# Both products of the first MLP as seven block products in chunks of 768 tokens, with p kept in DRAM between

## What is computed

```python
scores = scale * np.matmul(q, k.transpose(0, 1, 3, 2))          # masked to the window, softmax
x = np.matmul(attn, v)                                          # 2304 x 512
a = x @ w1; b = x @ w2                                          # 512 -> 1024 each
h = a * b @ w3; x = h @ w_out                                   # 1024 -> 1024 -> 512
h = x @ w_in; g = np.maximum(0.01 * h, h); out = g @ w_out2     # 512 -> 2048 -> 512
```

## Time and profile before

| | us |
|---|---|
| median of 3 runs (lowest, highest) | 795.57 (795.39, 797.1) |
| the profiled execution | 795.03 |
| its span, first to last instruction | 793.2 |
| TensorE busy | 775.2 |
| VectorE, ScalarE, GpSimd busy | 406.3, 374.5, 132.8 |
| HBM traffic | 155.74 MB, 195 GB/s over the span |

### The profile page before, as it was taken

The page is one execution under the profiler, slowest core; times in us unless marked ns, Lnnn a source line. Parts: engine busy times, 40 slices in busy tenths (PEclk is TensorE's granted clock), DMA queues, the critical chain, the costliest instruction groups (busy, mean ns, idle before and its releaser), DMA issues. The chain is left out here.

```text
span 793.2 us, 12523 instructions
## 1 busy us (share of the span) xinstructions
PE 775.2 (98%) x4944; PEld 751.5 (95%) x4944; DVE 406.3 (51%) x582; ACT 374.5 (47%) x814; POOL 132.8 (17%) x129
## 2 busy tenths in 40 slices
PE   6999999999999999999999999999999799999998
PEld 5788999999999999999999999999999699999998
DVE  4775442442443343333255577659778555445451
ACT  4775441442442343343235666456668454444441
POOL 0110450542451111111114005105100000000000
PEclk9999999999999999999999999999999999999999
DMA  7976462663563232221602675764999997768731
GB/s 276 325 248 220 159 224 97 230 258 129 208 236 113 86 118 97 83 87 34 239 1 81 237 267 193 265 224 161 359 356 339 321 315 250 217 189 245 212 95 60
DMA packets 65050, 155.74 MB, mean 196 GB/s; under 512 B 5344, under 2 KB 32992, under 8 KB 64992
## 3 DMA queue, kind: packets, MB, share of 16 engines
q1 hardware_dynamic: 55968, 137.12, 51.2%
q10 hardware_dynamic: 9024, 17.83, 5.9%
HBM read 104.07 MB, written 50.86 MB: 195 GB/s over the span
## 5 line engine op out<-in xcount | busy, mean ns | idle before, releaser
L287 PE MATMUL acc<-parts,weights_a 128*128 128x384 f32 x488 | 166.2, 341 | 0.4 <-DVE weights_b L873 0.4
L289 PE MATMUL acc<-parts,weights_a 128*128 128x384 f32 x488 | 163.2, 335 | 0.0
L288 PE MATMUL acc<-parts,weights_a 128*128 128x384 f32 x488 | 163.2, 334 | 0.0
L922 DVE TENSOR_TENSOR parts<-arena,parts 128x768 fp32r<-128x768 f32 x72 | 68.6, 958 | 66.0 <-ACT parts L726 65.9
L726 ACT ACTIVATE parts<-arena 128x768 fp32r<-128x768 f32 x72 | 60.5, 847 | 73.4 <-PE acc L289 25.8
L287 PE MATMUL acc<-weights_b 128*128 128x384 f32 (+1 forms) x256 | 93.3, 364 | 1.6 <-DVE weights_b L873 0.9
L287 PEld LDWEIGHTS acc<-parts,weights_a 128*128 128x128 f32 x488 | 91.7, 188 | 0.8 <-issue 0.8
L288 PEld LDWEIGHTS acc<-parts,weights_a 128*128 128x128 f32 x488 | 91.8, 188 | 0.0
L289 PEld LDWEIGHTS acc<-parts,weights_a 128*128 128x128 f32 x488 | 91.6, 188 | 0.0
L288 PE MATMUL acc<-weights_b 128*128 128x384 f32 (+1 forms) x256 | 90.0, 352 | 0.0
L289 PE MATMUL acc<-weights_b 128*128 128x384 f32 (+1 forms) x256 | 89.9, 351 | 0.0
(11 more groups left out here) (185 smaller groups left out, 1613.1 us busy)
## 6 DMA issues: line engine op xcount, KB each, us to landing
arena<-g_between SPq DMA_DIRECT2D x84, 384.0 KB, 4.1
g_between<-arena SPq DMA_DIRECT2D x24, 960.0 KB, 5.1
arena<-qkm_steps SPq DMA_DIRECT2D x36, 576.0 KB, 4.5
arena<-v_steps SPq DMA_DIRECT2D x36, 256.0 KB, 3.9
g_between<-arena SPq DMA_DIRECT2D x24, 384.0 KB, 6.1
arena<-wprod_tiles SPq DMA_DIRECT2D x16, 512.0 KB, 4.3
weight_sums<-arena ACTq DMA_DIRECT2D x16, 512.0 KB, 3.2
arena<-weight_sums SPq DMA_DIRECT2D x16, 512.0 KB, 5.6
```

Source lines behind the costliest of these rows:

```text
L287: eng.matmul(out_ap, w_hi, m_hi, start=start, stop=False, skip_group_check=resumed)
L288: eng.matmul(out_ap, w_hi, m_lo, start=False, stop=False, skip_group_check=resumed)
L289: return eng.matmul(out_ap, w_lo, m_hi, start=False, stop=stop, skip_group_check=resumed)
L922: dve.tensor_tensor(b[:, BW:2 * BW], t_raw[traw_slot(k)], b[:, 0:BW].bitcast(F32), ALU.subtract).then_inc(t_lo, 1)
```

## The change

The first MLP takes the form of the second. The order on TensorE is now:

- The first stage, with 12 attention steps instead of 6. `hu_sums` on POOL and `split_hu` on ACT and DVE make, in each of the 16 slots, one half of a unit of w1 and w2 with its sums (7 x 128 columns). wsum is copied out of PSUM and stored to DRAM.
- The rounds AB: 12 rounds of 14 slots in the order `AB_SEQ`. A slot (r, i, s) is product i for branch s (s = 0 is a, s = 1 is b), 6 matmuls of 384 columns. p's four blocks are products of two SBUF tensors (`make_p11`, `make_p22`, `make_p12`) or of PSUM and SBUF (`make_p21`); their sums follow (`p_sums`), and three stores take all to `pt_dram`. The other 24 attention steps lie in rounds 0 to 6 (`SCORES`); the values are copied by DVE instead of ACT.
- y: `y_product` for three chunks, seven products of two blocks `ty` each, blocks loaded through a ring of five places (two until k = 8).
- The second MLP as before, at other addresses.

The weight sums of w_in and w_out (`presums`, `load_pre`, `store_pre`) now start behind the last attention step, and their stores are issued by SP. wsum's units are summed and split by DVE and ACT in rounds 9 and 10 (`WSUM_SPLIT`). The mask comes once and not with every step. The diff, cut to its core:

```diff
+AB_SEQ = []
+for _r in range(AR):
+    AB_SEQ += [(_r, P1, 0), (_r, P1, 1)]
+    if _r == 0:
+        AB_SEQ.append((_r, P5, 0))
+    AB_SEQ += [(_r, P5, 1), (_r, P2, 0), (_r, P6, 0), (_r, P6, 1), (_r, P2, 1), (_r, P7, 0), (_r, P7, 1),
+               (_r, P3, 0), (_r, P3, 1), (_r, P4, 0), (_r, P4, 1)]
+    if _r + 1 < AR:
...
+AB_PAIR = (0, 1, 2, 3, 0, 1, 2, 3, 2, 3, 0, 1)
...
+SCORES0 = (-1, 0, 1, 2, 4, 5, 6, 7, 8, 9, 10, 11)
+TURN0, VALUES0 = 2, 3
...
+        SCORES[(_c + 1) * CSTEPS + _j] = slot_of(4 * _c, 2 + (33 * _j + 5) // 10)
+EXPS_A, EXPS_B, RECIP, TURN, VALUES = 2, 3, 4, 5, 8
...
+WSUM_SPLIT = {(9, 3): 0, (9, 8): 1, (10, 4): 2, (10, 9): 3}
+TY_FIRST = {3: 0, 5: 1, 9: 2, 12: 3}
...
+            def store_p(r):
+                c, jj = r // ROUNDS, AB_PAIR[r]
+                sp.wait_ge(p22_done, r + 1)
+                sp.wait_ge(pt3_made, r + 1)
+                sp.dma_start(pt_dram[c, 0:3, :, jj].rearrange("b p t -> p b t"), pa_st[:, :]).then_inc(p_stored[0], 16)
+                sp.wait_ge(pt1_made, r + 1)
+                sp.wait_ge(pt2_made, r + 1)
+                sp.dma_start(pt_dram[c, 3:5, :, jj].rearrange("b p t -> p b t"), pb_st[:, 0:2]).then_inc(p_stored[1], 16)
+            def store_p_late(r):
+                c, jj = r // ROUNDS, AB_PAIR[r]
+                sp.wait_ge(c21_done, 2 * r + 2)
+                sp.wait_ge(pt4_made, r + 1)
+                sp.dma_start(pt_dram[c, 5:7, :, jj].rearrange("b p t -> p b t"), pb_st[:, 2:4]).then_inc(p_stored[2], 16)
             def load_pre(u):
-                if u >= 2:
+                if u < 2:
+                    sp.wait_ge(values_done, NSTEP)
+                    sp.wait_ge(masked, NSTEP)
+                else:
                     sp.wait_ge(pre_stored[u % 2], u // 2 * 16)
-                elif u == 1:
-                    sp.wait_ge(piece_lo, NFIRST)
...
+            def store_pre(u):
+                sp.wait_ge(pre_s3, u + 1)
+                sp.wait_ge(pre_made, u + 1)
+                sp.dma_start(sums_dram[u], pre_raw[u % 2][:, QW:5 * QW]).then_inc(pre_stored[u % 2], 16)
...
+            def load_ty(k):
+                c, i, jp = k // (NPROD * JPY), k // JPY % NPROD, k % JPY
+                if i == 0 and jp == 0:
+                    for n in range(3):
+                        sp.wait_ge(p_stored[n], 16 * ROUNDS * (c + 1))
+                if TEARLY <= k < TEARLY + TRAWY - SPARE:
+                    sp.wait_ge(p_stored[k - TEARLY], 16 * AR)
+                if TY_BEFORE[k] is not None:
+                    sp.wait_ge(ty_lo, TY_BEFORE[k] + 1)
+                sp.dma_start(ty_raw[TY_SLOT[k]].rearrange("p (j t) -> p j t", j=2),
+                             pt_dram[c, P_AT[i], :, 2 * jp:2 * jp + 2]).then_inc(ty_in[TY_SLOT[k]], 16)
...
+                if r > 0 and n == slot_of(r, 2):
+                    store_p(r - 1)
+                    store_p_late(r - 1)
+            for u in range(2):
+                load_pre(u)
+            for r in range(8, AR):
+                store_p(r - 1)
+                store_p_late(r - 1)
+                if r == 8:
+                    load_wsum(0)
+                    load_wsum(1)
+                for u in range(3 * (r - 8), 3 * (r - 8) + 3):
+                    store_pre(u)
+                    load_pre(u + 2)
+                if r == 9:
+                    load_wsum(2)
+                    load_wsum(3)
+                if r == 10:
+                    load_ty(0)
+                    load_ty(1)
+            load_ty(2)
+            load_ty(3)
+            load_ty(4)
+            store_p(AR - 1)
+            load_ty(5)
+            store_p_late(AR - 1)
+            for k in [6, 8, 7] + list(range(9, TBY)):
+                load_ty(k)
+                if k == 8:
+                    store_pre(12)
+                    load_pre(14)
+                if k == 10:
...
+            def hu_sums(h):
+                a11, a12, a22, s4, s2, a21, s1 = [hu_raw[h % 2][:, q * P:(q + 1) * P] for q in range(NPROD)]
+                pool.wait_ge(hu_in[h % 2], 32 * (h // 2 + 1))
+                if h >= 2:
+                    pool.wait_ge(hu_lo, h - 1)
+                pool.tensor_tensor(s1, a21, a22, ALU.add).then_inc(hu_s1, 1)
+                pool.wait_ge(hu_s1, h + 1)
+                pool.tensor_tensor(a21, a11, a21, ALU.subtract).then_inc(hu_s3, 1)
+                pool.tensor_tensor(s2, s1, a11, ALU.subtract).then_inc(hu_s2, 1)
+                pool.wait_ge(hu_s2, h + 1)
+                pool.tensor_tensor(s4, a12, s2, ALU.subtract).then_inc(hu_made, 1)
...
+            def split_wsum(j):
+                act.wait_ge(wu_s3, j + 1)
+                act.wait_ge(wu_made, j + 1)
+                act.wait_ge(prod_done[P4], 2 * (9 + j // 2))
+                act.activation(units[HALF_UNITS + j][:, 0], wsum_raw[j % 2], ACT.Copy).then_inc(wu_hi, 1)
+            def split_ty(k):
+                if k < NPROD:
+                    act.wait_ge(prod_done[k], 2 * AR)
+                else:
...
+                    save_wsum(0)
+                    store_wsum(0)
+                for g in range(CSTEPS):
+                    if SCORES0[g] == k - 1:
+                        exps(g, range(HP))
+                split_hu(k)
...
+            for k in range(TROUND, TBY + NPROD):
+                c, i, step = (k - NPROD) // (NPROD * JPY), (k - NPROD) // JPY % NPROD, (k - NPROD) % JPY
+                r = YR0 + c
+                if k < TBY:
+                    split_ty(k)
+                else:
+                    split_x(NC2, XS_POS[k - TBY])
+                if k in Y_UNIT_SPLIT:
+                    split_unit(Y_UNIT_SPLIT[k])
+                if k >= NPROD and step == JPY - 1:
+                    for s in range(2):
+                        if i == P1:
+                            copy_p1(r, s)
...
+            def make_p11(r):
+                dve.wait_ge(c11_done, 2 * r + 2)
+                if r == 0:
+                    for m in range(2, 4):
+                        dve.wait_ge(wsum_stored[m], 32)
+                else:
+                    dve.wait_ge(p_stored[0], 16 * r)
+                dve.tensor_tensor(pa_st[:, 0], p1_sb[:, 0], p1_sb[:, 1], ALU.mult).then_inc(p11_done, 1)
+            def make_p22(r):
+                dve.wait_ge(c22_done, 2 * r + 2)
+                dve.tensor_tensor(pa_st[:, 2], p5_sb[:, 0], p5_sb[:, 1], ALU.mult).then_inc(p22_done, 1)
+            def make_p12(r):
+                dve.wait_ge(c12_done, 2 * r + 2)
+                dve.tensor_tensor(pa_st[:, 1], u2_sb[:, 0], u2_sb[:, 1], ALU.mult).then_inc(p12_done, 1)
+            def p_sums(r):
+                dve.wait_ge(p11_done, r + 1)
+                dve.wait_ge(p12_done, r + 1)
+                if r == 0:
+                    for m in range(2):
+                        dve.wait_ge(wsum_stored[m], 32)
+                else:
+                    dve.wait_ge(p_stored[1], 16 * r)
+                dve.tensor_tensor(pb_st[:, 0], pa_st[:, 1], pa_st[:, 0], ALU.subtract).then_inc(pt1_made, 1)
+                dve.wait_ge(p22_done, r + 1)
+                dve.wait_ge(pt1_made, r + 1)
+                dve.tensor_tensor(pa_st[:, 1], pa_st[:, 2], pa_st[:, 1], ALU.subtract).then_inc(pt3_made, 1)
+                dve.tensor_tensor(pb_st[:, 1], pa_st[:, 2], pb_st[:, 0], ALU.subtract).then_inc(pt2_made, 1)
+            def make_p21(r):
+                dve.wait_ge(c21_done, 2 * r + 1)
+                dve.wait_ge(prod_done[P4], 2 * r + 2)
+                if r > 0:
+                    dve.wait_ge(p_stored[2], 16 * r)
+                dve.tensor_tensor(pb_st[:, 2], bank(r, P4, 1)[:, 0:CT], p1_sb[:, 0], ALU.mult).then_inc(c21_done, 1)
+                dve.wait_ge(c21_done, 2 * r + 2)
+                dve.wait_ge(pt2_made, r + 1)
+                dve.tensor_tensor(pb_st[:, 3], pb_st[:, 2], pb_st[:, 1], ALU.subtract).then_inc(pt4_made, 1)
+            def wsum_sums(j):
+                a11, a12, a22, s4, s2, a21, s1 = [wsum_raw[j % 2][:, q * QW:(q + 1) * QW] for q in range(NPROD)]
+                dve.wait_ge(wu_in[j % 2], 32 * (j // 2 + 1))
+                dve.tensor_tensor(s1, a21, a22, ALU.add).then_inc(wu_s1, 1)
+                dve.wait_ge(wu_s1, j + 1)
+                dve.tensor_tensor(a21, a11, a21, ALU.subtract).then_inc(wu_s3, 1)
+                dve.tensor_tensor(s2, s1, a11, ALU.subtract).then_inc(wu_s2, 1)
+                dve.wait_ge(wu_s2, j + 1)
+                dve.tensor_tensor(s4, a12, s2, ALU.subtract).then_inc(wu_made, 1)
+            def split_wsum(j):
+                dve.wait_ge(wu_hi, j + 1)
+                u = units[HALF_UNITS + j]
+                dve.tensor_tensor(u[:, 1], wsum_raw[j % 2], u[:, 0].bitcast(F32), ALU.subtract).then_inc(wu_lo, 1)
+            def split_ty(k):
+                dve.wait_ge(ty_hi, k + 1)
+                b = block_places[k % NPROD]
+                dve.tensor_tensor(b[:, BW:2 * BW], ty_raw[TY_SLOT[k]], b[:, 0:BW].bitcast(F32),
+                                  ALU.subtract).then_inc(ty_lo, 1)
...
```

(94 more changed lines are left out.)

1571 lines of the change are left out of this document (847 added, 724 removed).

## The result

The changed kernel takes 893.79 us (median of four runs, 891.6 to 896.06); the kernel before took 795.48 us beside it. The ratio is 1.1233, with a 95% interval of 1.1199 to 1.1267: slower by 12%. The forecast said slower, but by 1.1%. The profiled execution has a span of 891.5 us, so 137.7 us were added to the ideal 753.8 of the forecast, where 49.1 had been expected.

What follows compares the result with a forecast made beforehand. TensorE's instruction count was taken to set the end, with starvation at hand-overs through DRAM. Ideal 753.8 plus 49.1 of stalls gave a span of 802.9, plus 1.8 made 804.7, stated as 804.5 us (1.1% slower), range 785 to 819.

Steps and rivals of the forecast that it cites:

- ideal 753.8: Whole span with nothing waiting: 793.2 less 37.4 for matmuls and 2.0 for first-stage waits, 753.8 us.
- count (37.4 us): First MLP on TensorE: 216 fewer matmuls at 0.1733 us each, saving 37.4 us.
- First stage: Twelve attention steps in 16 slots: ordered ACT and DVE queues add 6 us (0 to 12), AB starting near 85.
- turn of 5.6 us: First stage: mask, exponentials, both splits and values copy form a closed chain of 5.6 us; TensorE needs 4.9.
- Round 0 and attention rounds: AB rounds 0 to 7: late bank copy and turn add 4, late transposes and POOL beside DVE add 6 us.
- Round 8: AB round 8, between attention rounds and rounds 9 to 11: no added time expected, 0 us.
- Rounds 9 to 11: Last AB rounds: late p stores behind weight-sum units on SP, and wsum splits holding DVE, add 15.4 us (8 to 20).
- SP chain: Weight-sum units on SP between p stores and y's loads, each waiting for store landings, delay p and y's blocks.
- Start of y: First y chunk: late block loads, two ring places and copy_p1 behind split_ty(7) and (8) add 17.5 us (6.3 to 22).
- First products: Second MLP's first products: old code from there on, its 1.6 us kept, nothing added.
- A: Rival, whole kernel: the gain arrives because stalls absorb each other, 778 us; chance 0.24 for everything below 794.
- D: Rival, rounds 8 to 11 and y's start: POOL's 51 us of weight sums slow DVE, adding 15, 820 us; chance 0.17.

Runs made afterwards that it cites:

- turn6: Changed kernel with the transposes and values of each attention step in the AB rounds one slot later; 881.7 us.
- hu_late: Changed kernel with split_hu on ACT and DVE moved one slot later, to the start of the next turn; 884.4 us.
- all: Changed kernel with hu_late, turn6, pool_later, save_wsum ahead of the splits it stood behind, and weight-sum DMAs on POOL's queue with loads in pairs; 852.91 us.
- pool_later: Changed kernel with POOL's last sum of x and three splits held until DVE made the last product or sum of that chunk; 881.12 us.
- floor: Queue orders of all2 without its later places for weight units and without the weight sums (output not the reference's); 805.71 us, kernel before 794.69.
- no_pre: Changed kernel without the weight sums, their loads and stores; units take their places from the weights, so output isn't the reference's; 862.68 us.
- all2: Run all plus p1_first, weight-product-sum splits spread over rounds 9 to 11, and first four weight units loaded and split later in y; 841.95 us.
- p1_first: Changed kernel with ACT copying y's first product (copy_p1) ahead of split_ty(7); 890.71 us.
- stalls: Kernel before, with TensorE held back by POOL operations ahead of rounds 2, 6 and 10 of the first products; 817.94 us.
- pre_pool: Changed kernel with loads and stores of the 16 weight-sum units moved from SP's queue to POOL's; 907.62 us.

## Why the prediction was wrong

The direction was right, as were the count (37.4 us), the ideal lengths (round 1 in turn6: 23.10 for 23.1) and the second products. The places were mostly right too. The sum was wrong by 88.6 us, because nearly every term was sized too small, and all in the same direction:

- **First stage, 6 for 20.5.** The turn of 5.6 us was right for the first half (slots 2 to 7 start 5.2 to 5.9 us apart), but behind the middle they start 4.9 to 5.2 us apart. Hiding the split inside it gave back 7.3 us (hu_late), near the 6 of the forecast. What failed was the place of the copies of the accumulators in the queues: 9.9 us by the timeline, of which the forecast had 1.3. Taking them first gave back 4.3 (AB at 88.1 in all, 92.4 in hu_late). Each instruction between a stage's last matmul and the first use of its banks had to be looked at.
- **Round 0 and attention rounds, 9.7 for 35.1.** The forecast had the late turn, once by 2.4 us in round 0 and two or three times by 2 us after it. `normalize` on POOL was late in 15 of 24 steps, three times by over 2 us (3.4, 2.2, 2.2); one slot more recovers 15.7 us (turn6), of which 8.8 were waits. Round 4 adds 3.9 us by POOL beside DVE (pool_later). The other 15 us, of which floor still has 14, were not taken apart by a run. In floor's trace 8.4 of the 14 are seven waits, the longest 1.96 us (P5 of rounds 4 and 8 on `make_c12`), and 3.5 are pairs at the lower clock.
- **Round 8, 0 for 8.5.** The x splits for the third chunk meet DVE's sums there; 6.3 us went with pool_later. The forecast had the mechanism from the earlier trace rows, but named it for the attention rounds alone, without a price, and not for the place where a bank waits behind it.
- **Rounds 9 to 11, 15.4 for 24.7.** The waits stood where they were forecast: 1.7 us on `copy_u2`, 4.6 on `make_c12` of round 9, 4.9 on `make_p21` of round 10. The SP chain was there too, and later and slower than priced: the first weight sum began 13.2 us into round 8 and not 5.8, and a store took 5.1 us instead of the 3.2 of the earlier trace rows. Without weight sums 15.6 remain (59.3 for 43.7, no_pre), so about 9 are theirs; the order of the wsum splits is worth 4.7 (all against all2).
- **Start of y, 18 for 35.6.** That SP's chain makes y's blocks late was right; `load_ty(2)` was issued 7.3 us after y's start instead of 1.9, `load_ty(7)` 27 us after it instead of 19.5. That `copy_p1` behind the splits of ty decides was wrong (p1_first: the wait fell by 8 us, y by 3). The load of a block took 6.1 us, not 4.1, and 4.8 without the weight sums (no_pre). The formula of the Trainium skill (DMA: Bandwidth & Descriptors, Anatomy of one DMA) that the forecast set beside it is a fit for DMAs that GpSimd issues, and these loads are SP's. Without weight sums y costs 13.0 more than the ideal (no_pre), so they cost some 23.
- **First products, 0 for 13.6.** "From there on the code is the old one" was not so on POOL. In the kernel before the last sum of x2 has a place of its own (`extra`) and is made before the sums of g. In the kernel after it is made in place, waits for ACT's copy of P6, and so runs, with the three splits, beside all four sums of g at the ends of rounds 3 and 7: 2.60, 2.09, 2.60 and 2.09 us, where they take 0.95 and 0.56 alone. In the kernel before one of the four was free of it in round 3 and two in round 7. pool_later took 9.7 of the 13.6 away.
- **A term that was missing.** The clock: 25.8 us in pairs of matmuls at 1.2 GHz, against none before. A wait of 3 to 8 us costs 1.7 to 2.4 more behind it (stalls). With some 105 us of waits in many places this was a term as large as any other. The Trainium skill (TensorE: Matmul & The Clock Gate, Part 1) puts the penalty of the ramp at under 1% of a typical span, which it says of a kernel's start; here, with many ramps, it is 3%, and the measurement decides.

Of the rivals, A (stalls absorb each other) failed: there were 88.6 us more of them than forecast. pool_later shows that a little of it is true: of 19.8 us saved in four rounds the span kept 12.2. D, POOL beside DVE, was the right mechanism, but it was placed wrongly. DVE's operations in rounds 9 to 11 and in y are together only 3.5 and 1.3 us longer with the 256-column weight sums than without them (no_pre). It was the 768-column sums and splits of x at the chunk borders, 19.8 us by pool_later. Rival and forecast were not exclusive either; they should have been added. The range took the terms for independent, but they share, as I read it, one cause of error: each stall was priced for queues that are otherwise on time.

Open: about 2 of the 14 us above the ideal of rounds 0 to 7 in floor, and whether the weight sums fit beside the attention steps. That wasn't tried: their staging lies in memory that the attention still uses.

## What to carry to other kernels

Before trading matmuls for additions and round trips through DRAM, list for every stage border what must be done between the last matmul of a bank and its next use, on every engine's queue, and price the queue's worst turn, not its average: here the other engines were 25 to 59% busy, and the kernel came out 12% slower. Give the late chains (here weight sums of 8 us each, sixteen in a row) a place where nothing waits for their end. And add to every expected wait of TensorE of three microseconds and more about 2 us for the clock.

## What the runs showed of the hardware

- A wait of TensorE of 3.3, 5.4 or 8.3 us is followed by matmuls at 1.2 GHz that cost 1.7, 2.4 and 2.1 us more: in these three the surcharge hardly depends on the length of the wait. Shorter waits went either way: behind one of 2.9 us in the kernel before there is no slow matmul, behind one of 2.2 (at 156.1 us) in the kernel after there are. Over a whole kernel with many waits it reached 25.8 of 891.5 us.
- A DVE addition of 384 columns with both operands in SBUF takes 0.55 us alone and 1.9 to 2.0 beside a POOL operation of 768 columns, ending 0.41 us after it; with one operand in PSUM it stays at 0.55.
- The same store of 512 KB landed in a median of 3.2 us from ACT's queue (before), 3.2, 3.7 and 4.3 from POOL's (pre_pool, all, all2) and 5.1 from SP's, between other transfers. What of it is the queue and what the traffic was not separated. A load of 384 KB took 6.1 us in y, and 4.8 with the weight sums' transfers gone.
